# Last stretch of attention with two MLPs: first raw weight tiles, batch statistics and the product with g_ln moved in the order of work

## Reference

```python
# attention: keep the 32 largest scores of each row
scores = q @ k.T / sqrt(64);  kth = 32nd largest of the row
attn = softmax(where(scores >= kth, scores, -1e9));  x = attn @ v      # -> (4, 576, 512)
# first MLP, after a Fourier transform over tokens and width
u  = x + real(fft(fft(x, axis=1), axis=2))
un = (u - mean(u)) / sqrt(var(u) + 1e-6)
x  = u + relu(un @ w_ch1) @ w_ch2
# second MLP
xn = (x - mean(x)) / sqrt(var(x) + 1e-6) * g_ln
out = x + relu(xn @ w_ch1') @ w_ch2'
```

## Time and profile before

| | us |
|---|---|
| median of 3 runs | 1442.15 |
| lowest, highest | 1435.09, 1444.38 |
| profiled execution, its own time | 1436.72 |
| its span | 1434.8 |
| mean granted TensorE clock | 0.959 |
| busy PE / DVE / ACT / POOL | 1280.9 / 1137.8 / 776.8 / 348.3 |

### The profile page before, as it was taken

The page is one execution under the profiler, slowest core; times in us unless marked ns, Lnnn a source line. Parts: engine busy times, 40 slices in busy tenths (PEclk is TensorE's granted clock), DMA queues, the critical chain, the costliest instruction groups (busy, mean ns, idle before and its releaser), DMA issues.

```text
span 1434.8 us, 22757 instructions
## 1 busy us (share of the span) xinstructions
PE 1280.9 (89%) x7944; PEld 1044.2 (73%) x7944; DVE 1137.8 (79%) x2305; ACT 776.8 (54%) x1489; POOL 348.3 (24%) x305
## 2 busy tenths in 40 slices
PE   5777878799898799889988989999999999999999
PEld 3444544677677678777876778878688999989898
DVE  8999999789999998899889889965475455555544
ACT  4776663567677455564654556653444444344442
POOL 3433320112122241131233322231103020121210
PEclk7998899999999899999999999999999999999999
DMA  7899992456557655676665466663144343333342
GB/s 253 301 337 340 319 335 70 155 196 205 193 179 248 221 193 178 250 245 223 228 230 215 159 226 233 228 208 133 59 162 147 119 153 118 128 122 118 118 154 81
DMA packets 116530, 279.05 MB, mean 194 GB/s; under 512 B 29633, under 2 KB 29634, under 8 KB 116418
## 3 DMA queue, kind: packets, MB, share of 16 engines
q1 hardware_dynamic: 104658, 230.40, 47.3%
q10 hardware_dynamic: 10368, 42.47, 7.8%
q0 software_dynamic: 1392, 4.73, 1.1%
HBM read 234.30 MB, written 42.73 MB: 193 GB/s over the span
## 4 chain that ended last, share of the span: by engine, by line
PE 57%; DVE 29%; DMA 5%; issue 4%; ACT 2%; SPq 1%; POOL 1%; ACTq 0%; DVEq 0%
PE Big L717 23%; PE Big L700 15%; DVE top L1074 12%; DVE wk L1086 11%; PE Sp L700 7%; DMA wf<-in_weights 5%; DVE ex L1093 3%; PE Tp L648 2%; PE Tp L671 2%; PE Sp L744 2%; PE Sp L756 1%; PE Tp L665 1%; PE Tp L775 1%; PE Sp L606 1%; DVE nmx L1081 1%
## 5 line engine op out<-in xcount | busy, mean ns | idle before, releaser
L717 PE MATMUL Big<-wr,hh 128*128 128x512 f32 x1152 | 365.7, 399 | 0.0
L700 PE MATMUL Big<-uh,wr 128*128 128x384 f32 (+1 forms) x1376 | 316.7, 320 | 18.2 <-ACT hh L936 16.7
L1074 DVE MAX8 top<-wk 128x8 f32<-128x576 f32 x432 | 304.5, 746 | 0.0
L700 PEld LDWEIGHTS Big<-uh,wr 128*128 128x128 f32 x1376 | 233.7, 193 | 38.1 <-issue 30.3
L717 PEld LDWEIGHTS Big<-wr,hh 128*128 128x128 f32 x1152 | 220.6, 191 | 42.5
L717 PE MATMUL Big<-wr,hl 128*128 128x512 f32 x576 | 240.1, 417 | 5.3 <-DVE wr L1225 4.8
L482 POOL TENSOR_TENSOR hl<-hf,hh 128x256 fp32r<-128x256 f32 (+1 forms) x120 | 104.6, 871 | 502.1 <-ACT hh L936 502.0
L700 PE MATMUL Big<-ul,wr 128*128 128x384 f32 (+1 forms) x688 | 214.9, 312 | 0.0
L1086 DVE MATCH_REPLACE8 wk<-top,wk 128x576 f32<-128x576 f32 x288 | 211.6, 742 | 0.0
L648 PE MATMUL Tp<-ident,ex 128*128 128x128 f32 x720 | 120.0, 292 | 68.2 <-DVE ex L1093 54.2
L648 PEld LDWEIGHTS Tp<-ident,ex 128*128 128x128 f32 x720 | 88.2, 148 | 111.2 <-issue 66.0
(11 more groups left out here) (134 smaller groups left out, 1869.7 us busy)
## 6 DMA issues: line engine op xcount, KB each, us to landing
wf<-in_weights SPq DMA_DIRECT2D x204, 512.0 KB, 4.1
wr<-w_low SPq DMA_DIRECT2D x240, 256.0 KB, 4.2
sc<-in_weights SPq DMA_DIRECT2D x52, 512.0 KB, 3.2
sc<-sc_ahead ACTq DMA_DIRECT2D x36, 576.0 KB, 5.6
w_low<-wr SPq DMA_DIRECT2D x32, 512.0 KB, 6.4
sc_ahead<-U ACTq DMA_DIRECT2D x18, 576.0 KB, 5.4
sc_ahead<-un ACTq DMA_DIRECT2D x9, 576.0 KB, 3.6
sc_ahead<-yb ACTq DMA_DIRECT2D x9, 576.0 KB, 6.6
```

The costliest lines, as they stand in the source:

```text
L700: last = nc.tensor.matmul(hidden(n), a[:, kd * P:(kd + 1) * P], x[:, kd, 0:P * SIZE[p]], start=(kd == 0 and j == 0), stop=(kd == KD - 1 an ...
L717: last = nc.tensor.matmul(Ac[:, j, :], a[:, n % 2, j * P:(j + 1) * P], w, start=(f == 0 and m == 0), stop=(f == KF - 1 and m == 2))
L1074: nc.vector.max(top[:, s % RING, r, :], src).then_inc(s_top, 1)
```

## The change

Three moves, all of instructions that exist already.

1. SyncE issues the raw loads of tiles 120 and 121 when ACT has rounded w2 of tile 117 and of tile 118, the last users of these two buffers, and no longer of tile 119. Tiles 122 and 123, in the score buffer, now wait for tile 119 explicitly.
2. DVE's statistics of batch 3 come three slots after the combination they belong to: slots 154, 155 and 156, behind unit and split_w1_low.
3. For groups whose statistics come after the attention part (`ready_pair(p) >= PAIRS`; with a gain these are 9, 12 and 13) POOL's product with g_ln comes one slot sooner, in START-6 on.

```diff
+def gain_slot(p):
+
+    return START[p] - (6 if ready_pair(p) >= PAIRS else 5)
...
                 elif r >= 2:
                     sp.wait_ge(s_masked, TILES)
+                    sp.wait_ge(s_w2h, UP)
                 else:
-                    sp.wait_ge(s_w2h, UP)
+                    sp.wait_ge(s_w2h, n - WFS + 1)
                 sp.dma_start(raw(n), w_raw[tile_index(n)]).then_inc(s_wraw[r], 16)
...
                 for p in range(GROUPS):
-                    if ORDER[p][0] == 1 and 0 <= s - (START[p] - 5) < SIZE[p]:
-                        gain(p, s - (START[p] - 5))
+                    if ORDER[p][0] == 1 and 0 <= s - gain_slot(p) < SIZE[p]:
+                        gain(p, s - gain_slot(p))
...
                 for j in range(J):
                     if s == piece_slot(B - 1, 4 + 2 * j) + 1:
-                        combined(B - 1, j)
+                        combine(B - 1, j)
+                    if s == piece_slot(B - 1, 4 + 2 * j) + J + 1:
+                        own_stats(B - 1, j)
```

## The result

| | before | after |
|---|---|---|
| median of 11 runs each, us | 1441.78 | 1431.45 |
| lowest, highest | 1435.09, 1444.38 | 1425.22, 1435.89 |
| ratio, 95% interval | | 0.9925 (0.9905 to 0.9944) |
| span of the profiled execution | 1434.8 | 1429.6 |

What follows compares the result with a forecast made beforehand. The prediction took DVE to bound the attention part and PE the last stretch, where only PE's waits could be won. 1.8 + 2.5 + 5.6 = 9.9 us off the median 1442.15 gave 1432, 80% from 1425 to 1438.

Steps and rivals of the forecast that it cites:

- part 2: Statistics of batch 3 leave slots 151 to 153 for 154 to 156: gain 2.5 us (1.5 to 3.0).
- Part 1: Raw tiles 120 and 121 load sooner, so PE's wait for pT at 972 us goes: 1.8 us (1.1 to 1.8).
- early landing: Raw tile 120 lands 3.8 us after its issue, at 968.8, gaining the whole 1.78 us of PE's wait.
- Statistics 0: DVE's statistics after combination 0 of batch 3: hidden by 1.91 us of DVE idle time, so removal gives nothing.
- statistics 1: DVE's statistics after combination 1, on the path to PE's 4.75 us wait: removal takes 1.42 us off, leaving 3.3.
- no fall: PE keeps the full clock behind its gap at mlp2(129): the statistics move gains 3.0 us.
- short fall: PE runs 3.4 us at half clock behind the gap, losing 1.7 while DVE catches up 0.6: gain 1.9 us.
- Part 3: POOL's product with g_ln one slot sooner in groups 9, 12, 13 removes PE's waits: 3.6 + 1.0 + 1.0 = 5.6 us.
- The rule on POOL and VectorE: Shared SBUF interfaces: the moved product stretches both low halves, losing up to 0.7 us in group 9; total gain 9.2.
- (b): Contention wins or the wait is replaced: part 3 gives 4.2 or less, or long half clock; total 5 to 7; 17%.
- (d): Slower: moved statistics stall PE in slots 154 to 158, a DVE slot reaching over 5 us; 1448 us; 3%.
- (c): More than 1% faster, over 14 us: clock drops fall elsewhere, or run spread of 9 us adds; 11%.

Runs made afterwards that it cites:

- part 2 alone: The kernel before with only the statistics of batch 3 moved three slots behind their combination; stretch from the w_low DMA to the end 466.9 us against 470.1.
- the adds above: Changed kernel with POOL's adds of group 7's result held back until DVE has done combination 1 of batch 3; last stretch 461.3 us against 460.2.

## Why the prediction was right

The forecast was 1432, the measured median 1431.45; the sum 9.9, the trace's stretch 10.0. The three mechanisms were right. That the sum fits to a tenth is in part luck: part 2 gave 2.5 in this execution and 1.5 in the next of the same kernel.

- **Part 1, 1.8 forecast, 1.85 measured.** The early landing held: issue 0.36 behind the w_low DMA, no wait of ACT. That the DMA of 256 KB ahead costs nothing was a choice between bounds; ACT came to the tile 4 us after its issue, and nothing was left to see.
- **Part 2, 2.5 forecast, 2.48 measured, but one of its terms was a midpoint between cases and not a case.** Statistics 0 hidden, statistics 1 worth 1.4, gap 3.3 (3.36): shown by the rows. The new waits were set at 1.2, 0.3 of it combination 2's and 0.9 the statistics'; part 2 alone shows 1.0, 0.45 and 0.55. The clock I had halved between "no fall" (3.0) and "short fall" (1.9); the executions showed 3.0, 2.5 and 1.5. The short fall came, and cost less than I said because DVE's new waits vanished in it wholly and not by half: 1.4 of the gap and 1.1 of the clock make the 2.5. So this term came out right by chance.
- **Part 3, 5.6 forecast, 5.55 measured** (3.62, 0.97, 0.96). A turn without a wait for un costs 3.25 and 4.64, as the slots of the kernel before had said. That DVE's unit would just fit the 3.25 also held. I had counted six waits for un; the table of waits has four, of 1.76, 1.41, 0.49 and 0.49. What the third turn slots of groups 12 and 13 lost, 0.26 each, is seen in the spacing alone.
- **The rule on POOL and VectorE.** In its new place the second product stands beside w2 low of its slot, which took 1.04 in place of 0.69 (1066.92), not both low halves twice as long; the slot stayed at 2.81 (136 to 140 takes 11.23 in both kernels). So it cost nothing here, and 4.9 for part 3 was too low. That the two engines slow each other agrees with the rows: see the adds above.
- **Rivals.** (b), contention or a replacing wait: part 3 gives none; the long half clock of part 2 is real, in one of the two profiled executions of the changed kernel, and takes 1.0, not 3 to 5. (d), slower: tripled statistics reach the DVE slot of over 5 us that it named (1.55 + 1.4 + 2.4, measured 5.3 in two slots) and cost 5.4, of which 1.7 is a second fall of the clock; the statistics at their true length cost 0.55, so the rival needs three times the load in more slots than there are. (c), more than 1% by chance: 1425.22 and 1435.89 are both runs of the changed kernel, and the medians are 0.7% apart (the interval of the ratio, 0.56 to 0.95%, lies inside 1%).

## What to carry to other kernels

Measure a change at the end of a long program from an event that it can't move: here the untouched part alone varied by 8 us between executions, while behind it two executions of the changed kernel differed by 1.0, all of it the clock in one place. When an in-order engine serves another, put the short piece that is waited for ahead of the long one, and put work with no date where the served engine's slots are longest. For a wait, list what stands between it and its cause in the waiting engine's queue; where a third engine's transfer or copy sits there, moving one issue frees it.

## What the runs showed of the hardware

- **One gap, three outcomes.** PE was idle for 3.36 to 3.37 us between dense matmuls in five executions. One had no change of clock, three (among them the first of the changed kernel) had 3.4 us at 1.2 GHz, and one, the second of the changed kernel, had 6.8 us. With 4.75 idle it was 6.8 us in three of three, but 0.9, 1.0 and 2.8 us of it lay within the gap. Shorter waits did it too: the clock fell for 3.4 us behind a wait of 2.24, and behind two of 1.95 and 2.02 close together. In the two executions whose longest wait here was 1.45 it did not fall.
- **POOL beside VectorE.** POOL's product of 128x512 with g_ln takes 1.3 alone and 1.7 where it began while DVE's two-input operation ran; ul beside the same kind of operation took 1.3 to 1.45. DVE's two-input operations, where they lie wholly beside POOL, take 1.3 to 1.8 in place of 0.69, and 1.4 to 1.5 in place of 0.42 for 257 columns. Of hl with 256 columns, whose first input is in PSUM, no row beside POOL in the stretches read here is longer than 0.43. This is the rule of the Trainium skill (GPSIMD Engine Reference, Key points) with the sizes that this case gives.
